# Fused gated linear attention and four-expert layer: the third expert's tile groups ahead of the reloaded expert, attention units started in other slots, two wide steps with another order of products

## The reference

```python
C = f_stab * C + i_stab * outer(vt, kt)          # per head, step by step
n = f_stab * n + i_stab * kt
y[t] = sigmoid(o_gate) * (C @ qt) / max(|n . qt|, 1)

x = y.transpose(0, 2, 1, 3).reshape(1536, 320)
p = domain_probs / (domain_probs.sum(-1) + 1e-9)
for e in range(4):
    out += p[:, e:e+1] * (relu(x @ w1[e]) @ w2[e])
```

## Time and profile before

| | |
|---|---|
| executions | 413.1, 412.14, 412.25 us; median 412.25 us |
| the profiled execution's own time | 412.83 us |
| its span, first to last instruction | 410.9 us |
| TensorE (PE) busy | 403.0 us, 98% of the span, 2650 matmuls |
| VectorE (DVE) busy | 261.8 us, 64% |
| ScalarE (ACT) busy | 192.0 us, 47% |
| GpSimd (POOL) busy | 193.2 us, 47% |
| mean granted TensorE clock | 0.996 of full speed |
| moved by DMA | 54.48 MB, 133 GB/s over the span |

### The profile page before, as it was taken

One profiled execution on the slowest core, in us unless ns is written; L12 is line 12 of the kernel. 1 busy time (PEld: TensorE's weight loads), 2 busy tenths in 40 slices (PEclk: granted clock), 3 DMA queues, 4 the chain that ended last, 5 costly groups with the idle time before them and its releaser, 6 DMA issues.

```text
span 410.9 us, 7284 instructions
## 1 busy us (share of the span) xinstructions
PE 403.0 (98%) x2650; PEld 389.8 (95%) x2650; DVE 261.8 (64%) x490; ACT 192.0 (47%) x378; POOL 193.2 (47%) x227
## 2 busy tenths in 40 slices
PE   8999999999899999999999999999999999999997
PEld 8899999999899999999999999979999999999997
DVE  5885786759444538346249893668665666667654
ACT  4575478659242548434125442344553345434420
POOL 4865835487940558821602001567435643556300
PEclk9999999999899999999999999999999999999999
DMA  7889929684970606341016002222012211230002
GB/s 265 283 283 391 381 92 346 234 284 159 369 274 2 225 2 228 116 176 48 2 30 140 0 2 83 85 84 85 12 73 83 83 29 57 83 101 17 0 2 96
DMA packets 18052, 54.48 MB, mean 133 GB/s; under 512 B 2177, under 2 KB 8850, under 8 KB 16866
## 3 DMA queue, kind: packets, MB, share of 16 engines
q1 hardware_dynamic: 17442, 52.63, 36.8%
q10 hardware_dynamic: 576, 1.40, 1.0%
HBM read 50.40 MB, written 2.05 MB: 128 GB/s over the span
## 4 chain that ended last, share of the span: by engine, by line
PE 94%; DVE 4%; issue 1%; ACT 0%; POOL 0%; DVEq 0%
PE acc_ps L1611 21%; PE hid_ps L1592 21%; PE acc_ps L1677 16%; PE out_ps L1548 5%; PE hid_ps L1677 3%; PE acc_ps L1592 2%; PE out_ps L1655 2%; PE out_ps L1656 2%; PE out_ps L1654 2%; PE out_ps L1653 2%; PE out_ps L1555 2%; PE hid_ps L1441 1%; PE score_ps L1492 1%; PE score_ps L1655 1%; PE add_ps L1655 1%; PE add_ps L1656 1%
## 5 line engine op out<-in xcount | busy, mean ns | idle before, releaser
L1149 DVE SCALAR_TENSOR_TENSOR h_lo<-hid_ps,h_hi 128x384 fp32r<-128x384 f32 (+1 forms) x70 | 35.9, 513 | 84.6 <-ACT h_hi L809 84.3
L809 ACT ACTIVATE h_hi<-hid_ps 128x384 fp32r<-128x384 f32 (+1 forms) x70 | 31.8, 455 | 108.6 <-PE hid_ps L1592 108.5
L1611 PE MATMUL acc_ps<-w_hi,h_hi 128*128 128x320 f32 x208 | 66.4, 319 | 2.5 <-DVE y_acc L1169 2.2
L1611 PE MATMUL acc_ps<-w_hi,h_lo 128*128 128x320 f32 x208 | 64.4, 310 | 0.0
L1611 PE MATMUL acc_ps<-w_lo,h_hi 128*128 128x320 f32 x208 | 64.2, 308 | 0.0
L1592 PE MATMUL hid_ps<-xt_hi,w_hi 128*128 128x384 f32 (+1 forms) x210 | 57.1, 326 | 0.1
L1592 PE MATMUL hid_ps<-xt_hi,w_lo 128*128 128x384 f32 (+1 forms) x210 | 56.6, 324 | 0.0
L612 POOL TENSOR_TENSOR w_lo<-w_raw,w_hi 128x384 fp32r<-128x384 f32 x40 | 45.1, 1131 | 23.5 <-ACT w_hi L795 23.4
L682 POOL TENSOR_TENSOR w_hi<-w_raw,w_hi 128x640 fp32r<-128x640 f32 x12 | 19.6, 1634 | 53.1 <-ACT w_hi L852 53.1
L1611 PEld LDWEIGHTS acc_ps<-w_hi,h_hi 128*128 128x128 f32 x208 | 39.5, 190 | 2.8 <-DVE h_lo L1149 2.7
L676 POOL TENSOR_TENSOR left_lo<-w_raw,left_hi 128x384 fp32r<-128x384 f32 x12 | 13.2, 1101 | 56.6 <-ACT left_hi L835 56.6
(11 more groups left out here) (251 smaller groups left out, 996.6 us busy)
## 6 DMA issues: line engine op xcount, KB each, us to landing
w_raw<-in_w_b SPq DMA_DIRECT2D x19, 704.0 KB, 7.3
w_raw<-in_w_s SPq DMA_DIRECT2D x12, 832.0 KB, 4.6
raw<-in_qk_s SPq DMA_DIRECT2D x8, 1024.0 KB
g_all<-g_dram SPq DMA_DIRECT2D x10, 512.0 KB, 6.9
kv<-in_kv_n SPq DMA_DIRECT2D x12, 352.0 KB, 6.1
q_pack<-in_q_p SPq DMA_DIRECT2D x10, 192.0 KB, 6.9
out_y<-y_acc SPq DMA_DIRECT2D x12, 160.0 KB, 1.8
carry<-g_dram SPq DMA_DIRECT2D x30, 60.0 KB
```

What stands on the lines that cost most here:

```text
L809: nc.scalar.activation(h_hi[:, M % RING, 0:cols], hid_bank(M)[:, 0:cols], ACT.Relu).then_inc(hid_hi, 1)
L1149: nc.vector.scalar_tensor_tensor(h_lo[:, M % RING, 0:cols], hid_bank(M)[:, 0:cols], 0.0, h_hi[:, M % RING, 0:cols].bitcast(fp32), ALU.max, ...
L1611: last = nc.tensor.matmul(acc_ps[t][:, 0:DM], x, w, start=(f == 0 and i == 0), stop=(f == NF - 1 and i == 2))
```

## The change

It does four things.

1. The groups of eight slots are put in another order. Groups 0 to 2 (expert 0 on tiles 0 and 1, expert 1 on tiles 0 to 3) stay. Then come expert 2's two groups of three tiles (slots 24 to 39), and the reloaded expert 0 on tiles 2 and 3 after them (slots 40 to 47); before, this group of two tiles had slots 24 to 31 and expert 2 had 32 to 47. Expert 3's four groups stay in slots 48 to 79. The sum of the slots' matmuls is the same.
2. `EARLY` falls from 32 to 24: `up` runs two slots ahead up to slot 21 and one ahead after that, so that slots 40 to 47 are slots of two tiles with `up` one ahead.
3. Units 5 to 10 get other first slots: 20, 26, 32, 36, 48, 52 in place of 22, 30, 34, 40, 46, 50. The slots of the casts and of the remainders of q and k follow.
4. Wide step 1 has its products in the order 1, 6, 7, 4, 2, 5, 3 with the second-weight products after the 2nd, 3rd, 4th and 6th, and wide step 11 in the order 1, 6, 5, 7, 4, 2, 3. Block 21 is then finished before block 11 in both. VectorE's and ScalarE's lists for steps 0 to 2 are rewritten to match; in the later steps the remainder `step_rest_low` stands ahead of the second scaling into `y_acc`.

```diff
--- before.py
+++ after.py
@@ -29,16 +29,16 @@
 LAG, FIRST = 2, 4
 EARLY_SPLITS = {M: [M + 4] for M in range(12)}
 
-LOADS = (0, 1, 0, 2, 3)
-GROUPS = ((0, 0, 2), (1, 0, 2), (1, 2, 2), (2, 2, 2), (3, 0, 3), (3, 3, 3), (4, 0, 3), (4, 3, 3), (4, 6, 3), (4, 9, 3))
+LOADS = (0, 1, 2, 0, 3)
+GROUPS = ((0, 0, 2), (1, 0, 2), (1, 2, 2), (2, 0, 3), (2, 3, 3), (3, 2, 2), (4, 0, 3), (4, 3, 3), (4, 6, 3), (4, 9, 3))
 SLOTS = NF * len(GROUPS)
 N_BLOCKS = NF * len(LOADS)
 N_PAIRS = N_BLOCKS // 2
-T0 = {2: 2, 3: 6, 4: 16, 5: 22, 6: 30, 7: 34, 8: 40, 9: 46, 10: 50, 11: 56}
-EARLY = 32
+T0 = {2: 2, 3: 6, 4: 16, 5: 20, 6: 26, 7: 32, 8: 36, 9: 48, 10: 52, 11: 56}
+EARLY = 24
 DN_FIRST, DN_END = 0, 28
-CAST = {4: (11, 12), 5: (16, 17), 6: (24, 25), 7: (28, 30), 8: (35, 37), 9: (41, 43), 10: (44, 47), 11: (51, 52)}
-SUB = {4: (13, 14), 5: (18, 19), 6: (26, 27), 7: (30, 32), 8: (37, 38), 9: (43, 45), 10: (46, 48), 11: (53, 54)}
+CAST = {4: (9, 11), 5: (16, 19), 6: (20, 23), 7: (28, 29), 8: (31, 34), 9: (43, 44), 10: (47, 49), 11: (51, 54)}
+SUB = {4: (13, 14), 5: (18, 19), 6: (23, 25), 7: (29, 30), 8: (34, 35), 9: (44, 46), 10: (49, 51), 11: (53, 54)}
 OPEN_IN = {3: (2,), 13: (4,), 14: (6,), 17: (8,), 18: (10,)}
 LATER_PAIRS = {12: 8, 14: 9, 16: 10}
 
@@ -52,6 +52,8 @@
 SUM_AT = 2 * DM + 4 * 256
 W_STEP = SUM_AT + 4 * 256
 ORDER = (1, 6, 5, 7, 2, 4, 3)
+SECOND_ORDER, LAST_ORDER = (1, 6, 7, 4, 2, 5, 3), (1, 6, 5, 7, 4, 2, 3)
+SECOND_DOWNS = (1, 2, 3, 5)
 LEFT = {1: 0, 2: 1, 4: 2, 5: 3, 6: 4, 7: 5, 3: 6}
 RIGHT = {1: 0, 2: 1, 3: 2, 5: 3, 6: 4, 7: 5, 4: 6}
 TURNED = {5: 0, 7: 1, 4: 2, 6: 3}
@@ -178,9 +180,19 @@
     return wide_evictions(p - 2, 1, min(i, pairs(p - 2) - 1))
 
 
+def order_of(t):
+
+    return {1: SECOND_ORDER, STEPS - 1: LAST_ORDER}.get(t, ORDER)
+
+
+def blocks_of(t):
+
+    return (21, 11, 12, 22) if t in (1, STEPS - 1) else (11, 21, 12, 22)
+
+
 def product_count(t, m):
 
-    return len(ORDER) * t + ORDER.index(m) + 1
+    return len(ORDER) * t + order_of(t).index(m) + 1
 
 
 def halves_of(t):
@@ -949,21 +961,25 @@
                     wide_relu(0, 21)
             keep_1(1)
             wide_relu(0, 12)
-            for t in range(1, STEPS):
-                if t > 1:
-                    keep_1(t)
+            own_highs(2)
+            sums_highs(2)
+            wide_relu(0, 22)
+            step_down_high(2)
+            wide_relu(1, 21)
+            wide_relu(1, 11)
+            keep_5(1)
+            wide_relu(1, 12)
+            wide_relu(1, 22)
+            for t in range(2, STEPS):
+                keep_1(t)
                 if t + 1 < STEPS:
                     own_highs(t + 1)
                     sums_highs(t + 1)
                 keep_5(t)
-                if t == 1:
-                    wide_relu(0, 22)
                 if t + 1 < STEPS:
                     step_down_high(t + 1)
-                wide_relu(t, 11)
-                wide_relu(t, 21)
-                wide_relu(t, 12)
-                wide_relu(t, 22)
+                for c in blocks_of(t):
+                    wide_relu(t, c)
 
 
         @block.vector
@@ -1286,6 +1302,7 @@
 
                 dve.wait_ge(product_done, product_count(t, 6))
                 dve.wait_ge(kept_1_done, t + 1)
+                wait_if(dve, whole_of[12], t)
                 n = width(t)
                 nc.vector.tensor_tensor(sum_2[:, 0:n], out_ps[:, 0:n], kept_1[:, 0:n], ALU.add).then_inc(sum_2_done, 1)
 
@@ -1401,23 +1418,36 @@
                 if M == 78:
                     wide_low(0, 11)
             add_12(0)
+            add_2(1)
             wide_low(0, 12)
-            for t in range(1, STEPS):
+            add_3(1)
+            sums_lows(2)
+            add_21(1)
+            wide_low(0, 22)
+            wide_low(1, 21)
+            wide_low(1, 11)
+            step_rest_low(2)
+            add_12(1)
+            wide_low(1, 12)
+            wide_low(1, 22)
+            for t in range(2, STEPS):
                 add_wide(t, 0)
                 add_2(t)
                 if t + 1 < STEPS:
                     sums_lows(t + 1)
+                    step_rest_low(t + 1)
                 add_wide(t, 1)
-                if t + 1 < STEPS:
-                    step_rest_low(t + 1)
-                if t == 1:
-                    wide_low(0, 22)
                 add_3(t)
                 add_wide(t, 2)
-                add_wide(t, 3)
-                wide_low(t, 11)
-                add_21(t)
-                wide_low(t, 21)
+                if t < STEPS - 1:
+                    add_wide(t, 3)
+                    wide_low(t, 11)
+                    add_21(t)
+                    wide_low(t, 21)
+                else:
+                    add_21(t)
+                    wide_low(t, 21)
+                    wide_low(t, 11)
                 add_12(t)
                 wide_low(t, 12)
                 wide_low(t, 22)
@@ -1733,11 +1763,13 @@
             for t in range(1, STEPS + 2):
                 ahead, behind = halves_of(t)
                 turns = [(half_of, i) for half_of in (ahead, behind) if half_of is not None for i in range(pairs(half_of[1]))]
+                at = SECOND_DOWNS if t == 1 else range(len(turns))
                 for n in range(8):
                     if t < STEPS and n < len(ORDER):
-                        product(t, ORDER[n])
-                    if n < len(turns):
-                        wide_down(*turns[n][0], turns[n][1])
+                        product(t, order_of(t)[n])
+                    if n in at:
+                        half_of, i = turns[at.index(n)]
+                        wide_down(*half_of, i)
 
 
 def kernel(**inputs):
```

## The result

| | before | changed |
|---|---|---|
| executions (us) | 413.1, 412.14, 412.25, 414.05 | 409.92, 408.93, 407.71, 407.85 |
| median | 412.68 | 408.39 |
| ratio of the times | | 0.9894, 95% interval 0.9859 to 0.9928 |

The change gains 4.3 us. The prediction had -4.5 and 407.7.

The account below looks back on a forecast made before the run. TensorE, busy 403.0 of 410.9 us, bounds the kernel, so only its few stalls can be won. Terms -4.3 - 0.3 - 0.4 + 0.5 = -4.5 take the median from 412.25 to 407.7 us; range 406.6 to 411.0.

Parts of the forecast that it names:

- The stall: First group of three tiles: TensorE's waits for VectorE's y_acc, slow first matmuls and low clock all go, -4.3 us.
- Due times: Slots 20 to 24: down(24) due at 85.5 us, VectorE's queue up to the evictions done by 84.
- The clock: After the stall at slot 32: granted clock of 0.51 from 106.03 us costs 1.53 us, which goes with the stall.
- a clock of 1.00 throughout: Whole run: a granted clock of 1.00 everywhere would show the prediction right; a window at 0.5 anywhere, wrong.
- Short waits in the slots: Slots: new waits of 0.1 for unit 5's scores, 0.2 in slots 40 to 47, 0.2 elsewhere, +0.5 us.
- 0 to 0.6, I take 0.2: Slots 40 to 47, two tiles with up one ahead: new wait of 0.2 us, as only 0.7 of slack is left.
- Wide step 1: 0.64 us wait for block 21 and slower start go (0.8); new waits around products 7, 4, 3 cost 0.5; net -0.3.
- Wide step 11: 0.24 us wait at 399.99 for block 21 goes, with the slower start after it, -0.4 us.
- Loads: SyncE's list: unit 6's scores data, its g_all rows and two weight pairs change places, costed at nothing.
- the rival built on them: Unit 6's g_all rows land late for ScalarE's decays in slot 25; 413.5 to 414 us at 15 us landing; chance 0.05.
- VectorE late again at slot 24: Slot 24: VectorE's queue 1.9 us late, time 411.5 us; chance 0.14, of which 0.12 partial and 0.02 in full.
- The stall only moves: Slots 40 to 47: a wait of 2 us and 1.5 of clock come back, 411.8 us, no change; chance 0.10.

Follow-up runs that it names:

- e5: Kernel before with one VectorE row, unit 7's first remainder (1.26 us), moved behind slot 31's evictions, its other remainder to slot 33: 409.99 us against 413.00, ratio 0.9940.
- e7: Changed kernel with eight small multiplications, each waiting for the one before, on VectorE ahead of slot 23's evictions: 412.98 us against 413.00 for the kernel before, ratio 1.0000.
- e8: Changed kernel with fourteen small multiplications, each waiting for the one before, on VectorE ahead of slot 23's evictions: 415.51 us against 413.00 for the kernel before, ratio 1.0069.
- e2: Kernel before with the new groups, loads, switch slot and unit tables alone, wide steps as before: 408.62 us against 412.97, ratio 0.9887.
- e10: Changed kernel with the first eviction of wide step 12 ahead of the last g_lo on VectorE: 407.46 us against 412.50 for the kernel before, ratio 0.9865.
- e9: The changed kernel run again, five executions, with a second trace: 408.11 us against 412.50 for the kernel before, ratio 0.9892.
- e4: Kernel before with the new groups, loads and switch slot alone, units' first slots, casts and remainders as before: 411.84 us against 412.97, ratio 0.9983.
- e12: Changed kernel with wide step 12's first eviction earlier and weight pairs 4 and 3 loaded earlier on SyncE's queue: 407.37 us against 412.50 before, ratio 0.9869.
- e6: Kernel before with unit 7's first remainder and slot 29's w_lo both moved behind slot 31's evictions on VectorE: 410.34 us against 413.00, ratio 0.9943.

## Why the prediction was right, point by point

**The stall (-4.3 predicted).** Right in mechanism. `y_acc` is no longer waited for, the clock is full there, and VectorE's list up to the evictions ends in time. e5, e7 and e8 show from both sides that this one engine's queue sets the wait: at slot 24 the two delays agree to 0.02 us on what there was to spare, at slot 32 one row of 1.26 us took 1.60 off. One reading was wrong: the 23 rows are not "on end", since `prob` among them waited 0.58 us for GpSimd. The size was low. The slots' stretch fell by 4.70, with nothing lost elsewhere, where this term had 4.3. By the starts of matmuls the two waits held TensorE up by some 2.4 and 0.55 us with their slow first matmuls, 0.2 more than I had, and another 0.3 went at 85.2 to 85.7, where the additions and their second matmul came late without a wait that the profile lists; no row of mine had that. Together these are the missing 0.4, within 0.1.

**Due times.** `down(24)` was put at 85.5 and started at 87.92, but that whole execution was 2.3 us later by slot 16 (65.01 against 62.73), so the laid-out time of slots 16 to 24 was right within 0.2. The 1.5 us to spare was 1.9.

**The clock (1.53 of the 4.3).** Confirmed in size where it is paid: 1.54 by e5, 1.61 and 1.39 by e7 and e8. The prediction assumed that the clock falls because of the stall and stays up without it. The second half holds for this place in every trace without the stall. The first half holds for 40 of 63 executions only, by their mean clock; in the other 23 the term is 0 as far as the mean tells, and the gain was 3.2 us in place of 4.7 (e2). The forecast did not consider that, and the medians hide it because more than half of the executions pay. The sign "a clock of 1.00 throughout" failed in the first trace, at 38.65, for a reason ahead of the change. See also the last section.

**Short waits in the slots (+0.5 predicted).** None came. From 50 to 264 us TensorE is busy in every one of 214 us. This is one of the two terms that were wrong in the slots; it and the 0.4 too little for the stall made -3.8 into -4.7. The scores of unit 5 (taken at +0.1) started without a wait. In slots 40 to 47 the cover was as thin as I had it:

```profile
152.22 1.92 DVE L1105 TENSOR_TENSOR split_qk<-raw,split_qk 40x1024 fp32r<-40x1024 f32 x1
154.16 0.42 DVE L1165 SCALAR_TENSOR_TENSOR h_lo<-hid_ps,h_hi 128x256 fp32r<-128x256 f32 x1
```

`down(46)` starts at 154.76, 0.18 behind the end of that `h_lo`. So of a slack of 0.7 a remainder of 1.92 us, longer than any in the earlier trace rows, took 0.5, and it still held. "0 to 0.6, I take 0.2" had the right lower end.

**Wide step 1 (-0.3 predicted).** Measured -0.44. The new waits are where they were put and smaller in sum. Products 7, 4 and 3, and the first `wide_down` of step 2, the first and the last with the matmul before them:

```profile
264.36 0.31 PE L1707 MATMUL acc_ps<-w_hi,h_lo 128*128 128x320 f32 x1
264.57 0.50 PE L1683 MATMUL out_ps<-t_hi,left_hi 128*128 128x512 f32 x1
...
266.55 0.50 PE L1683 MATMUL out_ps<-t_hi,left_hi 128*128 128x512 f32 x1
...
271.20 0.47 PE L1683 MATMUL add_ps<-xt_hi,left_hi 128*128 128x512 f32 x1
...
272.90 0.40 PE L1686 MATMUL score_ps<-rest,left_hi 96*128 96x512 f32 x1
273.13 0.46 PE L1707 MATMUL acc_ps<-w_hi,h_hi 128*128 128x320 f32 x2
```

Products 7 and 4 follow 0.21 behind a matmul of 320 columns (the one before product 4 starts at 266.34), where the pace is 0.147, and their own first matmul takes until 0.33 later in place of 0.23. With product 3, whose first takes 0.30, that is 2 x (0.06 + 0.10) + 0.07 = 0.4. I took 0.5. The 0.8 before `wide_down` of step 2 is gone: it follows 0.23 behind a matmul of 512 columns, which is the pace.

**Wide step 11 (-0.4 predicted).** The wait that I named is gone, but the stretch gained 0.05. What I did not look for is the next thing on VectorE's list: the evictions that free the banks for the second half. With the earlier wait gone, TensorE gets there before VectorE has done them, and loses 0.15 of waiting and about as much in slower first matmuls. e10 shows that the 0.40 was there, and comes once the eviction goes ahead of `g_lo`. This is the step of the prediction that was wrong in mechanism: a wait was costed as if nothing stood behind it.

**Loads (0 predicted).** Right. Unit 6's `g_all` rows were issued at 84.50, and ScalarE took them at 91.23 without waiting; the rival built on them did not occur.

**The sum.** -4.5 predicted, -4.3 and -4.4 measured, but by stretches -5.19. The misses (0.9 too little in the slots, 0.14 in step 1, 0.35 too much in step 11) do not cancel, and the first stretch makes up the rest: for the two profiled executions, 412.83 and 408.25, the times differ by 4.58, which is 5.19 less the 0.61 that e9's start took longer. That -4.3 and -4.4 lie so near the forecast is in part luck: by stretches the gain was 0.7 larger, and the slower start and the executions of the kernel before without the low clock hide it. The start took 0.6 us longer in e9 than before, and 2.3 in the first trace. The range has a slip too: the terms' best and worst ends as given add up to -5.2 and -3.4, not -5.5 and -3.2. On the start: kernels with the old unit tables had 62.65 to 63.00 there and once 63.44 (e4), those with the new ones 62.95 to 63.46 and once 65.01 (e12, with other loads, 62.55). Ahead of slot 16 the two programs differ in ScalarE's casts of unit 4, at slots 9 and 11 in place of 11 and 12, and in little else. Whether these cost some tenths or the executions merely fell so is open; it was not tried.

**The rivals.** VectorE late again at slot 24 did not happen. What it rests on showed itself all the same, in the 1.92 us above, while GpSimd's `w_lo` beside it took 1.86 in place of 0.88. There was room for it. By the Trainium skill, GPSIMD Engine Reference, Specifications, GpSimd and VectorE contend for SBUF when VectorE has two inputs there; the traces agree, see the last section. "The stall only moves" needs the unit tables to stay as they were, which is e4: it gained 0.7 (-1.5 to +0.1), where this rival said no change.

## What to carry to other kernels

When a hand-ordered kernel stalls, count the late engine's queue up to the instruction that is waited for and price the stall with the low clock that follows it: here one row of 1.26 us moved behind the evictions gave 2.8 us, 1.5 of them the clock's. Such a price is that of the traced execution: look at the mean clock of the others before taking it for all. When a wait is removed, read on along the same engine's list before booking the gain, since the next item in it is late by the amount that was won; here that took 0.35 of 0.40 at the end. When a row is moved, look at what it will run beside: in e6 the moved rows slowed GpSimd, and that took the whole of the second row's gain. And to measure changes smaller than the spread of executions, cut the traces at instructions that all kernels share: the stretches repeated to 0.01 us in the changed kernel, the medians to about one.
